# SyncE bounds how many weight pieces of the expert layer are underway

## The reference

```python
# x: 1536 tokens x 512, 8 experts, w1[e]: 512 x 1024, w2[e]: 1024 x 512
logits = x @ w_gate
expert_idx = np.argmax(logits, axis=1)
gate_w = softmax(logits)[token, expert_idx]
# each expert takes its tokens in order, up to `capacity` (384)
h = np.maximum(np.einsum('ecd,edf->ecf', disp, w1), 0.0)
y = np.einsum('ecf,efd->ecd', h, w2)
out[token] = gate_w[token] * y[expert of token, its place]
```

## Time and profile before

| | |
|---|---|
| median of 3 runs | 597.62 us (597.15 to 597.78) |
| profiled execution, its own time | 596.42 us |
| its span, first to last instruction | 594.7 us |
| mean granted TensorE clock | 0.995 |
| TensorE busy | 578.6 us, 97% |
| VectorE, ScalarE, GpSimd busy | 60%, 47%, 26% |
| weight pieces of the experts, median from issue to landing | 6.0 us |
| gathers, median from issue to landing | 6.4 us |

### The profile page before, as it was taken

How to read it: one execution, slowest core, us unless ns; L and a number is a source line. 1 busy time by engine, 2 the same in 40 slices (tenths; PEclk the granted TensorE clock), 3 DMA queues, 4 the chain that set the end, 5 groups by cost and what they waited for, 6 DMA issues and landing times.

```text
span 594.7 us, 11492 instructions
## 1 busy us (share of the span) xinstructions
PE 578.6 (97%) x3819; PEld 490.5 (82%) x3819; DVE 359.1 (60%) x1060; ACT 276.7 (47%) x683; POOL 157.0 (26%) x253
## 2 busy tenths in 40 slices
PE   8999999999999999999999999998999999999994
PEld 7787888888888888888888899886888888888883
DVE  5878786575556555765656446456745387499210
ACT  5866554333343335333433121124846497599320
POOL 5423542222111222223122200005203162354001
PEclk9999999999999999999999999999999999999998
DMA  7536443001062302010000060017955679599000
GB/s 196 145 94 175 141 109 82 8 19 39 19 177 71 89 19 72 19 37 19 37 0 19 5 209 1 1 38 225 335 201 165 227 244 389 171 364 335 18 21 19
DMA packets 73351, 67.70 MB, mean 114 GB/s; under 512 B 42900, under 2 KB 49060, under 8 KB 73280
## 3 DMA queue, kind: packets, MB, share of 16 engines
q1 hardware_dynamic: 68464, 57.50, 30.4%
q0 software_dynamic: 3760, 9.03, 5.0%
q10 hardware_dynamic: 1056, 0.26, 0.2%
HBM read 58.01 MB, written 12.06 MB: 118 GB/s over the span
## 4 chain that ended last, share of the span: by engine, by line
PE 87%; DVE 6%; ACT 3%; issue 3%; POOL 0%; DVEq 0%; POOLq 0%; ACTq 0%
PE bank L1067 22%; PE bank L1069 22%; PE bank L1068 22%; PE bank L1057 11%; PE bank L1111 4%; PE bank L1142 4%; PE bank L1215 1%; ACT wh L788 1%; DVE fw L1659 1%; DVE fw L1664 1%; DVE wl L1432 1%; DVE fw L1475 1%; DVE rw L1453 1%; ACT rw L800 1%; PE bank L1157 1%
## 5 line engine op out<-in xcount | busy, mean ns | idle before, releaser
L1067 PE MATMUL bank<-wh,rw 128*128 128x512 f32 x416 | 167.1, 402 | 1.8 <-DVE rw L1670 1.6
L1069 PE MATMUL bank<-wh,rw 128*128 128x512 f32 x416 | 163.1, 392 | 0.0
L1068 PE MATMUL bank<-wl,rw 128*128 128x512 f32 x416 | 162.8, 391 | 0.0
L1067 PE MATMUL bank<-rw,wh 128*128 128x256 f32 x384 | 112.7, 294 | 0.0
L1069 PE MATMUL bank<-rw,wl 128*128 128x256 f32 x384 | 108.5, 282 | 0.0
L1068 PE MATMUL bank<-rw,wh 128*128 128x256 f32 x384 | 108.1, 282 | 0.0
L935 ACT CAST rw<-fw 128x256 fp32r<-128x256 f32 x95 | 38.6, 406 | 142.8 <-DVE fw L1664 139.6
L1069 PEld LDWEIGHTS bank<-wh,rw 128*128 128x128 f32 x416 | 78.1, 188 | 17.2
L1067 PEld LDWEIGHTS bank<-wh,rw 128*128 128x128 f32 x416 | 78.3, 188 | 15.7 <-DVE rw L1670 2.2
L1068 PEld LDWEIGHTS bank<-wl,rw 128*128 128x128 f32 x416 | 78.4, 188 | 12.4
L1432 DVE TENSOR_TENSOR wl<-fw,wh 128x512 fp32r<-128x512 f32 x120 | 77.1, 688 | 9.4 <-ACT wh L788 6.7
(11 more groups left out here) (139 smaller groups left out, 697.5 us busy)
## 6 DMA issues: line engine op xcount, KB each, us to landing
fw<-in_moe_w_dram SPq DMA_DIRECT2D x95, 256.0 KB, 6.0
v_raw<-in_moe_w_dram SPq DMA_DIRECT2D x22, 256.0 KB, 6.0
fw<-in_moe_w_in_dram SPq DMA_DIRECT2D x16, 256.0 KB, 3.2
fw<-in_moe_w_out_dram SPq DMA_DIRECT2D x16, 256.0 KB, 2.8
y_scratch<-fw SPq DMA_DIRECT2D x12, 256.0 KB, 2.0
out_dram<-v_or_route SPq DMA_DIRECT2D x12, 256.0 KB, 3.4
v_raw<-in_v_dram SPq DMA_DIRECT2D x11, 256.0 KB, 3.3
o_sb<-in_q_dram SPq DMA_DIRECT2D x11, 256.0 KB, 3.2
```

The lines of the kernel that those rows point to most:

```text
L1067: pe.matmul(dst, ah, bh, start=start, stop=False, skip_group_check=True)
L1068: pe.matmul(dst, ah, bl, start=False, stop=False, skip_group_check=True)
L1069: return pe.matmul(dst, al, bh, start=False, stop=stop, skip_group_check=True)
```

## The change

In SyncE's last loop, from piece 15 on, a wait is added: before a piece is issued, the piece four before it must have landed. So at most four pieces are underway at a time. No instruction changes its place, and no DMA changes its size, source or buffer.

```diff
@@ -69,6 +69,7 @@
     STG = 4
     GRF, GR = 4, 5
     STGF, STG2 = 8, 11
+    UNDERWAY = 4
     AHEAD = 7
     NC = N // CW
     OPEN = AHEAD + NF - 1
@@ -574,6 +575,9 @@
 
             sp.wait_ge(y_stored, 16 * NT)
             for p in range(NP1 + STG2, NPALL):
+                if p > NP1 + STG2 + FIRST:
+                    _, _, _, _, landed, value = piece(p - UNDERWAY)
+                    sp.wait_ge(landed, value)
                 if p == NP1 + STG2 + FIRST:
                     sp.wait_ge(output_zeroed, 16 * NT)
                     sp.wait_ge(index_steps, NIX)
```

## The result

The change makes the kernel slower: 602.36 us, median of 8 runs (598.46 to 605.22), beside 597.4 us for the kernel before (596.24 to 597.82, 8 runs). The ratio is 1.0087, with 1.0057 to 1.0116 as its interval, about 5 us. The runs of the changed kernel also lie further apart: 6.8 us instead of 1.6.

The account below looks back on a forecast made before the run. TensorE, busy for 97% of the span and never waiting for a weight, was taken as the bound. Waits 0, late pieces 0 and freed waits 0 left the runs' median: 597.6 us, no change, range 596.8 to 599.0 us.

Parts of the forecast that it names:

- the three places named: Where ScalarE splits pieces as they land, with slacks to TensorE's need of 0.6, 1.8 and 2.2 us; no TensorE wait forecast.
- Place 2: Expert 0, pieces 25 to 31 split ahead of the hidden values: slack 1.8 us, lateness at most 0.6 us, no TensorE wait.
- The sign named for a wrong forecast: In expert 6's first tile, matmuls at the tenth place waiting for `wl` would show the forecast wrong.
- Does a window of four keep the DMA engines fed?: SyncE's loads: four underway give one piece per 0.66 us against the engines' 0.65, losing 0 to 0.06 us per piece.
- So over these stretches it isn't the limit.: At the tight places pieces already land 0.85 to 1.01 us apart; the window needs only 0.66 us per piece.
- The window starves the load: Slower rival: a piece takes 3.5 us under load, 0.91 us per piece; TensorE waits about 2 us, 599.6 us; chance 0.14.
- place 1: Start of expert 6, pieces 100 to 102: tightest slack, 0.6 us; lateness 0.2 us, at most 0.6, no TensorE wait.
- place 3: Expert 6, piece 117 split ahead of the hidden values: slack 2.2 us; lateness 0.3 us, at most 1.2, no TensorE wait.
- point of decision: The starving rival starts to cost at expert 6's start once a piece's way reaches between 2.7 and 3.9 us.
- fewer pieces in the queue: Faster rival: gathers and matmuls gain, 0.04 us on each of 28 matmul blocks, 1.1 us, 596.5 us; chance 0.05.
- what was to show the forecast right: Way about 3 us, SyncE waiting for landings, 370 GB/s in 435 to 438 us, TensorE busy, ScalarE's waits 4 to 7 us.
- The test named for a burst: A burst of loads at 330 GB/s or less would show the forecast wrong; 370 or more in 435 to 438 us, right.

Follow-up runs that it names:

- window_early: The window of four holds only for pieces 15 to 58, against the kernel before without a window: 597.61 us, ratio 1.0.
- window_4: The changed kernel itself, measured again in a later session against the kernel before: 602.82 us, ratio 1.0073.
- window_late: The window of four holds only from piece 59 on, against the kernel before without a window: 600.98 us, ratio 1.0068.
- four_reordered_b: Changed kernel, with expert 6's first-tile hidden values split before pieces 112 to 119, against the kernel before: 600.31 us, ratio 1.0042.
- window_3: At most three pieces underway in place of four, against the kernel before without a window: 612.59 us, ratio 1.0256.

## Why the prediction was wrong

**What bounds the kernel, and what counts.** Right: TensorE sets the pace, the change can only cost, and only where a piece eats the slack. Two of the three places named are where it stood. Place 2, in expert 0, did not: window_early costs nothing. The sign named for a wrong forecast came, a matmul at the tenth place of expert 6's first tile that waits for `wl` (536.92 us).

**"Does a window of four keep the DMA engines fed?"** This step failed. It took the 2.5 us of a piece in an idle queue as the way of a piece with three neighbours, and concluded (2.5 + 0.15)/4 = 0.66 us per piece. The same formula holds with what was measured, a mean way of 3.73 us alone and 0.02 us, not 0.15, from a landing to the next issue: (3.73 + 0.02)/4 = 0.94 us, which is what the middle of the phase shows. In the kernel the way is 4.2 us, which makes 1.05. The earlier trace rows had no piece with one to three neighbours, so the way between 2.5 us (idle) and 5.7 us (nine underway) was left open, and the end that suited was taken. The prediction even argued that the other number, 5.0 us, was gathers alone.

The trace of the kernel before did have the number, ahead of the experts, where the first weight pieces are issued into an idle queue. Issues of line 500 there, two and two of one burst of ten, and three at 400 us:

```profile
L500 SPq DMA_DIRECT2D fw<-in_moe_w_dram x2: 333/382/432, 340.6 to 340.9; - x2
...
DMA to landing us min/median/max: 2.7/2.9/3.0
...
L500 SPq DMA_DIRECT2D fw<-in_moe_w_dram x2: 432/432/432, 341.4 to 341.9; - x2
...
DMA to landing us min/median/max: 4.5/4.6/4.7
...
L500 SPq DMA_DIRECT2D fw<-in_moe_w_dram x3: 333/365/370, 400.1 to 401.0; - x3
...
DMA to landing us min/median/max: 2.7/2.9/3.6
```

The first two pieces took 2.7 and 3.0 us, the third and the fourth, with two and three ahead of them and more behind, 4.5 and 4.7 us; of the three at 400 us the last took 3.6 us. No gather ran beside the burst; at 400 us GpSimd issued one at 401.9 us, beside the last piece. By the prediction's own formula 3.6 to 4.7 us are 0.9 to 1.2 us per piece: enough to see that four don't feed the engines.

**The Trainium skill's rule.** The Trainium skill, "DMA: Bandwidth & Descriptors", "Where 436 GB/s comes from", would bind the loads at about 358 GB/s and so make the window free. The prediction set it aside for the 403 GB/s of its trace, and rightly: 512 KB pieces with eight underway move 377 GB/s over 31 us. But the window isn't free, as the rule would have it, and it isn't at the knee, as the prediction had it: four pieces move 279 GB/s, below either. The Trainium skill's fit in "Anatomy of one DMA" gives 2.6 us for a lone piece, an estimate worked out from its 2.0 us and 436 GB/s for DMAs of GpSimd's kind; the trace agrees for SyncE's (2.6 us with window 1). Among four it is 3.7 us, and the fit has no term for that.

**"So over these stretches it isn't the limit."** This failed too. The 0.85 to 1.01 us per piece of the earlier trace rows were averages that held the gathers' time and ran with a full queue. A window costs on top: beside gathers it is 1.18 us per piece (25.96/22), against 1.01 with eleven. In the kernel after, the nine pieces that end with number 100 landed in 11.3 us (522.5 to 533.8) instead of 9.1, and the 17 from 100 to 117 took 18.7 (533.83 to 552.56) instead of 14.5.

**The rival.** "The window starves the load" named the mechanism. Its sum for every piece stretched by 0.26 us, 1.7 us at place 1, 0.5 at place 2 and 2.2 at place 3, was 4.4 us; measured are 1.9, 0 and 2.3 us in the profile of the kernel after, and 1.8, 0 and 1.1 us in that of window_4. It halved that to 2 us for its 599.6, and left out two terms: the half clock (1.6 us in the one profile, none in the other) and the hidden values of expert 3 (1.2 and 2.3 us). Its point of decision, a way of 2.7 to 3.9 us, was right, and the measured 3.7 to 4.2 us lies at its upper end. What was wrong was its chance of 0.14: the way of a piece under load was the one number on which everything hung, and none of the rows chosen had it.

**The others.** Nothing was gained from fewer pieces in the queue: windows of six to ten are no faster than before. That the added waits themselves cost nothing is borne out to within 1.8 us. Of what was to show the forecast right, the way fell to 4.2 us and not to 3, and ScalarE's wait was 10.0 us and not 4 to 7. The test named for a burst was drawn in the right place. The stretch that it names and the whole burst of the kernel after, without gathers:

```profile
435.00:438.00 3.00, 3.00 (x15) 2.49 (x14) 2.06 (x4) 2.17 (x4) 0.00 (x0) 1.00 0.88 317
...
435.00:445.00 10.00, 10.00 (x48) 8.31 (x47) 2.66 (x4) 3.54 (x7) 0.00 (x0) 1.00 0.81 280
```

and the burst of the kernel before, which is over earlier:

```profile
425.00:437.00 12.00, 12.00 (x59) 10.03 (x58) 9.72 (x16) 8.88 (x16) 0.00 (x0) 1.00 1.03 379
```

317 GB/s is below the 330 that was to refute the forecast, and 280 GB/s (0.94 us per piece, as alone) stand against 379, though TensorE doesn't feel it there.

**Open.** Why the executions of the changed kernel spread over 7 us. The half clock doesn't sort them: the mean granted clock was 0.996 for the fastest run (598.46 us) and 0.990 for the slowest (605.22 us), but 0.986 for one of 601.72 us, and window_4's of 603.31 us had 0.996. Why the last of the 16 marks falls behind among four pieces is not shown either: it is only measured that it does. A window that goes on when half of the 16 marks are there wasn't tried.

## What to carry to other kernels

A limit on DMAs underway is to be priced with the time a DMA takes among as many others, never with the way of one in an idle queue; here 2.6 us became 3.7, and the window went from free to a quarter below the full rate (279 against 377 GB/s). Look for that time in the whole trace, also in stages that the change doesn't touch; here it stood in the first burst of the same loads. Where no row shows it, one small kernel with windows of 1 to 11 gives the whole curve, and the forecast should give the bad end its full chance. And lateness that an in-order engine takes in travels on: some two fifths of the cost (2.5 of 6.0 us by the medians of one chip) lay on hidden values of expert 6 that merely stood behind late splits, and moving them ahead gave it back.

## What was not expected of the hardware

- 256 KB loads need six underway to come near the full rate: in the middle of a phase four move 279 GB/s, six 366 and eleven 377. Over a phase of 22 it is 0.84 us each with six, 1.02 with four, 1.14 with three and 1.44 with two.
- The last of a load's 16 landing marks comes 0.5 us after the first when it is alone, and 1.2 us after it among four.
- SyncE's next issue starts 0.02 us after the landing that it waits for.
- Two 512 KB loads underway move 239 GB/s, four of 256 KB 264 GB/s, eight of 512 KB 377 GB/s, each over a phase of 11.5 MB.
- TensorE idle for 2.2 us amid an expert at full clock was followed by 3.4 us at the lower level, 1.6 us of cost; in window_late it was 2.3 us and then 3.4 us again, in four_reordered_b 2.2 us. In window_3 it was idle for 2.1 us until 511.7 us, in window_early for 1.9 us until 533.9 us, and the clock stayed at its full level.
